# Reordering the score slots of a pair of attention heads, with three and four score tiles in the two groups for ScalarE

## The reference

```
scores = scale * q @ k.T                   # 4 batches x 12 heads, 448 tokens, 64 dims
scores = cap * tanh(scores / cap)
attn   = exp(scores) / sum(exp(scores))    # the maximum cancels
x      = attn @ v                          # heads side by side: 4 x 448 x 768
# stage 2: theta = x @ w_theta; y = w_tok_r @ (x cos theta) + w_tok_i @ (x sin theta)
#          u = x + y;  u + relu(u @ w_ch)
# stage 3: token MLP (448 -> 256 -> 448) and channel MLP (768 -> 1536 -> 768)
```

## Time and profile before

| | us |
|---|---|
| profiled execution, device time | 897.8 |
| its span in the trace | 895.8 |
| PE busy | 870.3 (97%) |
| DVE busy | 450.3 (50%) |
| ACT busy | 306.1 (34%) |
| POOL busy | 193.9 (22%) |

### The profile page before, as it was taken

How to read it: one execution, slowest core, us unless ns; L and a number is a source line. 1 busy time by engine, 2 the same in 40 slices (tenths; PEclk the granted TensorE clock), 3 DMA queues, 4 the chain that set the end, 5 groups by cost and what they waited for, 6 DMA issues and landing times.

```text
span 895.8 us, 12482 instructions
## 1 busy us (share of the span) xinstructions
PE 870.3 (97%) x5164; PEld 736.3 (82%) x5164; DVE 450.3 (50%) x625; ACT 306.1 (34%) x355; POOL 193.9 (22%) x139
## 2 busy tenths in 40 slices
PE   8999999996799999999999999999999999999998
PEld 5445544496799999999999997888899988889998
DVE  5899999989868796724343443221400130003002
ACT  6989998744343443412121121111100100001000
POOL 0435535246333342261000013800000000000000
PEclk9999999999799999999999999999999999999999
DMA  7545674244211221230000134500210030002001
GB/s 172 163 132 152 165 192 116 59 114 104 61 50 49 62 62 36 105 112 1 1 1 1 63 100 138 177 1 0 73 69 1 1 106 1 1 0 71 1 1 53
DMA packets 57576, 61.96 MB, mean 69 GB/s; under 512 B 22288, under 2 KB 52912, under 8 KB 57520
## 3 DMA queue, kind: packets, MB, share of 16 engines
q1 hardware_dynamic: 57296, 60.94, 23.9%
q10 hardware_dynamic: 224, 0.23, 0.1%
HBM read 47.13 MB, written 14.02 MB: 68 GB/s over the span
## 4 chain that ended last, share of the span: by engine, by line
PE 87%; DVE 8%; issue 2%; ACT 1%; DMA 1%; SPq 0%; DVEq 0%; ACTq 0%
PE psum L1086 24%; PE psum L1088 24%; PE psum L1087 24%; PE psum L1128 7%; PE psum L1098 5%; PE psum L1103 2%; PE psum L1155 2%; PE psum L1236 1%; DVE wide_lo L960 1%; DVE tile_sums L807 1%; DVE reduced L914 1%; ACT wide_hi L712 1%; DMA kq_raw<-kq_t 0%; DVE reduced L910 0%; DVE tile_sums L815 0%
## 5 line engine op out<-in xcount | busy, mean ns | idle before, releaser
L1069 DVE SCALAR_TENSOR_TENSOR relu_lo<-psum,relu_hi 128x512 fp32r<-128x512 f32 (+1 forms) x48 | 30.0, 625 | 271.8 <-ACT relu_hi L776 271.8
L776 ACT ACTIVATE relu_hi<-psum 128x512 fp32r<-128x512 f32 (+1 forms) x48 | 26.2, 546 | 307.3 <-PE psum L1088 297.2
L1086 PE MATMUL psum<-wide_hi,mlp 128*128 128x512 f32 (+1 forms) x288 | 105.1, 365 | 2.2 <-DVE wide_lo L960 2.2
L1087 PE MATMUL psum<-wide_lo,mlp 128*128 128x512 f32 (+1 forms) x288 | 104.8, 364 | 0.0
L1088 PE MATMUL psum<-wide_hi,mlp 128*128 128x512 f32 (+1 forms) x288 | 104.7, 364 | 0.0
L1088 PE MATMUL psum<-relu_hi,mlp 128*128 128x512 f32 (+1 forms) x288 | 104.1, 362 | 0.0
L1087 PE MATMUL psum<-relu_lo,mlp 128*128 128x512 f32 (+1 forms) x288 | 104.1, 362 | 0.0
L1086 PE MATMUL psum<-relu_hi,mlp 128*128 128x512 f32 (+1 forms) x288 | 104.1, 362 | 0.0
L1128 PE MATMUL psum<-ring,values 128*32 128x448 f32 x768 | 81.4, 542 | 0.9 <-issue 0.9
L649 ACT ACTIVATE ring<-psum,score_scale 128x1792 f32<-128x1792 f32 (+1 forms) x48 | 75.2, 1567 | 17.6 <-PE psum L1155 8.8
L652 ACT ACTIVATE ring<-ring,cap_col 128x1792 f32<-128x1792 f32 (+1 forms) x48 | 77.1, 1606 | 1.6
(11 more groups left out here) (134 smaller groups left out, 1961.0 us busy)
## 6 DMA issues: line engine op xcount, KB each, us to landing
kq_raw<-kq_t SPq DMA_DIRECT2D x47, 224.0 KB, 3.7
mlp_raw<-moe_w_ch SPq DMA_DIRECT2D x24, 384.0 KB, 6.6
values<-v SPq DMA_DIRECT2D x48, 112.0 KB, 3.4
inverse_rows<-inverse_scratch SPq DMA_DIRECT2D x12, 448.0 KB, 6.0
rows_scratch<-turned SPq DMA_DIRECT2D x112, 48.0 KB, 1.7
x_rows<-rows_scratch SPq DMA_DIRECT2D x28, 192.0 KB, 2.4
u_scratch<-x_t SPq DMA_DIRECT2D x2, 1344.0 KB, 6.5
out_t<-x_t SPq DMA_DIRECT2D x4, 672.0 KB, 3.3
```

The source lines that it names most:

```text
L776: act.activation(relu_hi[c % 3][:, 0:n_tokens], psum[:, c % 2, 0:n_tokens], ACT.Relu).then_inc(relu_hi_made, 1)
L1069: dve.scalar_tensor_tensor(out=relu_lo[c % 3][:, 0:n_tokens], in0=psum[:, c % 2, 0:n_tokens], scalar=0.0, in1=relu_hi[c % 3][:, 0:n_tokens ...
L1086: pe.matmul(out, left[0], right[0], start=start, stop=False)
L1087: pe.matmul(out, left[0], right[1], start=False, stop=False)
```

## The change

The seven tiles are numbered A0, B0, A1, B1, A2, T, B2, and the groups for ScalarE are tiles 0 to 2 (A0, B0, A1) and 3 to 6 (B1, A2, T, B2). The slots of a score are (A0, B0), (A1, T), (A2, B1), (T, B2), where they were (A0, B0), (A1, B1), (A2, T), (T, B2). The wait for `tail_opened` stands between slots 2 and 3. As T belongs to group 1 and is written in slot 1, PE now waits for tanh of the previous pair's group 1 before slot 1 and not before slot 2. `SUMS_BANK` is 2, the bank of A1, and two banks of stage 2 change places with it. `weigh_first` issues one slot of values and `weigh_second` three. On DVE both additions wait for group 1, stand next to each other, and `copy_sums` comes behind them.

```diff
-A0, A1, B0, B1, A2, T, B2 = range(PAIR_TILES)
-GROUPS = ((0, 4), (4, PAIR_TILES))
-VALUES_BANK, SUMS_BANK = 7, 3
+A0, B0, A1, B1, A2, T, B2 = range(PAIR_TILES)
+GROUPS = ((0, 3), (3, PAIR_TILES))
+VALUES_BANK, SUMS_BANK = 7, 2
...
-        THETA_BANKS = (0, 1, 2, 3)
+        THETA_BANKS = (0, 1, 3, 2)
...
                 if pair >= 2:
                     dve.wait_ge(keys_summed, pair - 1)
-                dve.wait_ge(probs_ready, group_end(pair, 0))
+                dve.wait_ge(probs_ready, group_end(pair, 1))
...
                 dve.wait_ge(tiles_added, pair + 1)
-                dve.wait_ge(probs_ready, group_end(pair, 1))
                 dve.tensor_tensor(total, total, tiles_of_both(pair, A2, B2), ALU.add
...
                 add_first(pair)
+                add_second(pair)
                 if pair >= 1:
                     copy_sums(pair - 1)
-                add_second(pair)
                 copy_heads(pair)
...
-                    if step == 0 and a_tile == T:
-                        pe.wait_ge(tail_opened, pair + 1)
...
                 score_slot(pair, 0, A0, 0, B0, 1)
                 after(pe, sums_copied, pair - 2)
-                score_slot(pair, 1, A1, 1, B1, 2)
                 after(pe, tanh_done, group_end(pair - 1, 1))
-                score_slot(pair, 2, A2, 2, T, 0)
+                score_slot(pair, 1, A1, 1, T, 0)
+                score_slot(pair, 2, A2, 2, B1, 2)
+                pe.wait_ge(tail_opened, pair + 1)
                 score_slot(pair, 3, T, 3, B2, 3)
...
                 weigh_slot(pair, 0, V_A, A0, V_B, B0)
+
+            def weigh_second(pair):
+
+                pe.wait_ge(probs_ready, group_end(pair, 1))
                 weigh_slot(pair, 1, V_A + 1, A1, V_B + 1, B1)
-
-            def weigh_second(pair):
-
-                pe.wait_ge(probs_ready, group_end(pair, 1))
                 weigh_slot(pair, 2, V_A + 2, A2, V_B + 2, B2)
```

More of the change, by code:

```diff
@@ L1137, in weigh_first @@
                 weigh_slot(pair, 0, V_A, A0, V_B, B0)
-                weigh_slot(pair, 1, V_A + 1, A1, V_B + 1, B1)
             def weigh_second(pair):
                 pe.wait_ge(probs_ready, group_end(pair, 1))
+                weigh_slot(pair, 1, V_A + 1, A1, V_B + 1, B1)
                 weigh_slot(pair, 2, V_A + 2, A2, V_B + 2, B2)
```

## The result

The changed kernel takes 901.29 us (median of 20 runs, 895.79 to 904.14), the kernel before 896.90 (20 runs, 893.71 to 902.81): ratio 1.0041, 95% interval 1.0026 to 1.0056. It is slower by 4.4 us. That is within the range given (894.0 to 902.0), but outside the forecast's own (896.8 to 900), and of the three outcomes it is the one held second likeliest (0.35): the forecast was 898.5 and no measurable change. Measured again later, the same kernel was slower by 1.4 us only (see the end of the experiments). The profiled execution took 900.5, its span is 898.5, 2.7 above before.

What follows compares the result with a forecast made beforehand. PE's own work was taken to bound stage 1, with DVE nearly full behind it. Terms -6.7 + 6.5 + 1.6 = +1.4 put the profiled 897.8 at 899.2, or 898.5 us as a median; range 894.0 to 902.0.

Steps and rivals of the forecast that it cites:

- the three outcomes: Whole kernel against the kernel before: faster, chance 0.15; no measurable change, 0.50; slower, 0.35.
- T's stall goes, -6.7: PE, stage 1, slot 3: the stall at T's second write vanishes, 0.33 us per pair, period 6.88 to 6.55; -6.7 us.
- The first two scores yield nothing: PE, start of stage 1: scores 0 and 1 wait for tanh, so they gain 0 us from the removed stall.
- ACT costs nothing at 6.55: ACT, stage 1: groups are ready just in time at period 6.55, its floor being 6.19; cost 0 us.
- DVE: the limit goes from 1.59 to 0.60, +6.5: Stage 1: copy_heads may start only 0.60 us after a score's start, not 1.59, before PE is held; +6.5 us.
- The same sum: PE's wait per stage 1 burst: 0.2 + DVE's work - pairs x period - limit; 2.8 us before, 8.4 afterwards.
- The restarts: PE, stage 1: each wait for DVE's copy of sums costs 0.1 us more at restart; 9 waits, 0.9 us.
- The burst grows, +1.6: DVE beside GpSimd, stage 1: add_second directly behind add_first makes five pairs longer by 0.33 us each; +1.6 us.
- Stages 2 and 3 move with stage 1: Stages 2 and 3: they follow stage 1's last copies and shift with them; no term of their own.
- Rival 2: Stage 1: DVE becomes the bound, growth of 0.54 us on ten pairs; +5.2 us, 902.3 us; chance 0.32.
- rivals 1 and 3: Stage 1: first, DVE doesn't fall behind, 893.6 or 890.3 us, chance 0.15; second, T's stall stays, 902 us, 0.03.

Runs made afterwards that it cites:

- the hold: GpSimd starts its split of the last stage's third weight tile only after DVE made wide_lo: changed kernel 899.20 us, kernel before 896.25 us.

## Why the prediction was right or wrong

*T's stall goes, -6.7.* Right. Undisturbed periods are 6.53 (6.55 forecast), and without GpSimd's work the 21 periods are shorter by 144.08 - 137.11 = 7.0.

*The first two scores yield nothing.* Off by 1.4 in the profiled pair: the step looked at when each tanh ends, not at how long PE stands idle. Its wait grew from 1.5 to 2.1, and the clock fell behind it. With PE kept busy there the 1.4 is gone. But the loss is not shown to be the change's: with a wait of 1.5 as before, the clock also fell in the start of the two other profiles that have it (third score at 20.38 and 21.84), so that the 18.64 of before is the luckiest of three.

*ACT costs nothing at 6.55.* Right: ACT idles less than 0.1 in an undisturbed pair, and PE has no wait for ACT behind the third score.

*DVE: the limit goes from 1.59 to 0.60, +6.5.* Right, and the centre of the case. The same sum with the bursts of the changed kernel's own trace (7.70; 8.89; 21.91 for three pairs; 9.12; 17.37 for two) gives 0.77, 1.96, 1.92, 2.19 and 3.91, together 10.8; PE waited 10.4. One line of DVE's order moved back took 7 to 10 us off (each taken against before of its own session), the same line moved in the kernel before put 5 on. The restarts were put at 0.9 against none before; they were 0.7 against 0.3.

*The burst grows, +1.6.* In sum DVE's work did not grow: from the first copy of heads to the 23rd DVE was busy for 140.32, before for 140.82. What grew is the bursts that hold PE: the same sum gives 8.4 with the distances of before and 10.8 with those of the changed kernel, +2.4. Nor is it `add_second` alone: over the stretch of the bursts its mean rose from 1.21 to 1.33, the cast's from 0.89 to 1.19, and the means of the other two fell. That the cast is hit at all goes against the prediction's sentence that an instruction with at most one SBUF input takes no part. It leaves out a condition: the Trainium skill ("SBUF — State Buffer", Who interferes with whom) excepts DVE's 2-port modes there, which casts can enter. This case's cast, with one SBUF input, took 9.81 for 0.65 beside GpSimd's clearing; that it ran in such a mode no run here shows. The copies out of PSUM stayed at 0.61. Which operation a burst meets is chance.

*No term at all: the clock, +3.1 in the 21 periods.* The waits were summed as if a microsecond of waiting cost a microsecond. In the 21 periods of all profiles the granted clock fell to 0.50 at each of the ten waits of 2.05 to 3.74 (in seven profiles), for 3.4 us, once for 6.8, which cost 1.4 to 1.6 in most and 2.8 once; behind 1.92, 1.86 and 1.76 it stayed. No bound may be drawn from that: in the last stage it fell behind 1.84, in the start of two experiments at a wait of 1.68 (the 1.51 of PE's list) that in the profile of before cost nothing, and at the end of stage 1 with the copy ahead of both it stayed at 1.00 behind one of 2.37:

```profile
174.73 0.96 PE L1126 MATMUL psum<-ring,values 128*32 128x448 f32 x8 [2.37 <-issue]
```

How much of the 4.4 us this term makes in the median is open. It is clear in the profiled pair, but a profile of before with the hold has such a fall too, and in the repeat, where the change cost 1.4, the mean clock of the two kernels is the same.

*Stages 2 and 3 move with stage 1.* Right up to the last stage (everything is 5.5 to 6 later), where a race between DVE and GpSimd turned out another way in the profiled execution.

So with 1.4 and 3.1 for the clock in the sum, +1.4 would have been +5.9, which is what the profiled pair shows up to the last stage; the 3.3 that came back there is luck. Without the clock, the terms measured in stage 1 come to +1.3 (-7.0, waits +7.5, restarts +0.4, the last copy of heads +0.4), beside the forecast's +1.4. The mechanism of the forecast is thus shown, and the step that is missing in it is the price of the clock behind long waits. Rival 2 priced the outcome of the 20 runs (902.3) for a wrong reason (growth on ten pairs); rivals 1 and 3 did not come. The result lies in the stated range because that range takes in both neighbours of the forecast.

## What to carry to other kernels

When a stall is removed on the bounding engine, ask for each engine that feeds it how late it may be, and recompute that room after the edit: here the reorder spent 1.0 of the 1.6 us by which a copy could be late, on a queue that worked 129 of 141 us. In a queue, what someone waits for goes as early as its input allows and no earlier: between the additions was better by 6 us than ahead of both and by 7 to 10 than behind both. A few long waits of TensorE can cost more than many short ones of the same sum, since the clock may fall at them. And one pair of profiles can hold a lucky execution: compare the granted clock of each stage before putting a difference down to the change.

## What was not expected of the hardware

The price of a wait can appear behind it, on matmuls that work, and on no line of waits: steps of 0.37 for 0.20. When the fall comes varies: in the changed kernel 1.3, 1.2 and 0.2 us after the three waits ended, over all profiles up to 1.6 after the end, and in five of them once by 0.07 to 0.8 us before it (0.6 in the kernel with the old slots: 150.99 against 151.60). And where DVE and GpSimd hinder each other, a start 0.01 or 0.05 us to either side of the other's moved PE's work by over 2 us in the trace (`wide_lo` 5.05 or 3.36, GpSimd's split 1.84 or 5.01, and the clock behind it).
